# Order of weight splits and row preparation in an expert stage, and experts' weights read in 1 KB runs

## The reference

```
x = attention(x, state)                   # 8 batches x (512 + 32) tokens, 8 heads of 64: 4352 rows of 512
h = x @ w_in; x = (h * clip(h + 3, 0, 6) / 6) @ w_out          # 512 -> 2048 -> 512
logits = x @ w_gate; e_idx = argmax(logits, axis=1)
gate_w = softmax(logits)[e_idx]; eom = sigmoid(x @ w_output_gate)
for e in range(8):                        # w1[e]: 512 x 1024, w2[e]: 1024 x 512
    mask = e_idx == e
    out[mask] = gate_w[mask] * eom[mask, e] * (relu(x[mask] @ w1[e]) @ w2[e])
```

## Time and profile before

| | us |
|---|---|
| runs | 1163.8, 1163.85, 1164.52 |
| median | 1163.85 |
| the profiled execution's own time | 1164.95 |
| its span, first to last instruction | 1163.2 |

### The profile page before, as it was taken

How to read it: one execution, slowest core, us unless ns; L and a number is a source line. 1 busy time by engine, 2 the same in 40 slices (tenths; PEclk the granted TensorE clock), 3 DMA queues, 4 the chain that set the end, 5 groups by cost and what they waited for, 6 DMA issues and landing times.

```text
span 1163.2 us, 20924 instructions
## 1 busy us (share of the span) xinstructions
PE 1121.9 (96%) x6358; PEld 887.6 (76%) x6359; DVE 647.1 (56%) x1247; ACT 467.9 (40%) x781; POOL 76.8 (7%) x96
## 2 busy tenths in 40 slices
PE   9999999999999999999999988988899999989996
PEld 7777777777777777777778977867788888767885
DVE  6675654655646556556564347464465445446642
ACT  4454434443444344434544352442343223334420
POOL 0000100101001001010010110000101110000111
PEclk9999999999999999999999988989999999989998
DMA  9200110102001111020020275765676553765552
GB/s 365 91 37 8 66 37 37 44 30 74 37 6 68 37 37 41 33 74 1 1 110 1 104 252 179 244 208 176 218 236 208 163 160 117 243 203 177 178 155 63
DMA packets 98784, 131.37 MB, mean 113 GB/s; under 512 B 13967, under 2 KB 75023, under 8 KB 94352
## 3 DMA queue, kind: packets, MB, share of 16 engines
q1 hardware_dynamic: 91360, 89.35, 24.0%
q10 hardware_dynamic: 1584, 23.07, 5.9%
q0 software_dynamic: 5760, 17.90, 4.1%
HBM read 85.86 MB, written 45.47 MB: 113 GB/s over the span
## 4 chain that ended last, share of the span: by engine, by line
PE 80%; DVE 4%; DMA 4%; issue 3%; ACT 3%; SPq 3%; ACTq 2%; DVEq 0%; POOL 0%; POOLq 0%
PE y_ps L855 33%; PE h_ps L837 15%; PE y_ps L928 12%; PE h_ps L912 5%; PE y_ps L912 5%; DMA hid_mv<-hidden 3%; PE a_ps L812 2%; PE h_ps L827 2%; ACTq L444 2%; ACT we L1076 1%; DVE we L483 1%; SPq L574 1%; SPq L609 1%; PE a_ps L715 1%; PE a_ps L796 1%
## 5 line engine op out<-in xcount | busy, mean ns | idle before, releaser
L855 PE MATMUL y_ps<-w_out_hi,hid_hi 128*128 128x512 f32 x544 | 217.6, 400 | 0.0
L855 PE MATMUL y_ps<-w_out_hi,hid_lo 128*128 128x512 f32 x544 | 212.2, 390 | 0.0
L855 PE MATMUL y_ps<-w_out_lo,hid_hi 128*128 128x512 f32 x544 | 212.0, 390 | 0.0
L928 PE MATMUL y_ps<-we,act_t_hi 128*128 (+1 forms) x608 | 187.1, 389 | 1.2 <-DVE yo L1543 1.2
L1365 DVE SCALAR_TENSOR_TENSOR hid<-hid,h_ps 128x512 f32<-128x512 f32 (+1 forms) x144 | 94.4, 656 | 166.5 <-ACT hid L1035 166.5
L837 PE MATMUL h_ps<-att_hi,mix 128*128 128x512 f32 x512 | 184.0, 402 | 0.1
L1035 ACT ACTIVATE hid<-h_ps,three 128x512 f32<-128x512 f32 (+1 forms) x144 | 95.4, 662 | 174.9 <-PE h_ps L837 151.5
L855 PEld LDWEIGHTS y_ps<-w_out_hi,hid_hi 128*128 128x128 f32 x544 | 102.1, 188 | 50.0 <-issue 30.4
L1374 DVE TENSOR_TENSOR hid_lo<-hid,hid_hi 128x512 fp32r<-128x512 f32 (+1 forms) x144 | 94.8, 658 | 70.4 <-ACT hid_hi L1043 69.9
L928 PEld LDWEIGHTS y_ps<-we,act_t_hi 128*128 128x128 f32 x608 | 114.1, 188 | 25.2 <-issue 1.6
L912 PE MATMUL h_ps<-we,xg_t_hi 128*128 (+1 forms) x304 | 100.2, 413 | 22.8 <-DVE xg_t_lo L1419 11.5
(11 more groups left out here) (215 smaller groups left out, 1410.9 us busy)
## 6 DMA issues: line engine op xcount, KB each, us to landing
raw<-in_w ACTq DMA_DIRECT2D x11, 2048.0 KB, 8.3
hidden<-expert_hid SPq DMA_DIRECT2D x76, 256.0 KB
hid_mv<-hidden SPq DMA_DIRECT2D x152, 128.0 KB
xg<-buckets SPq DMA_DIRECT2D x164, 64.0 KB
xb<-in_x_rows SPq DMA_DIRECT2D x8, 1024.0 KB, 4.9
x_t<-in_x_t SPq DMA_DIRECT2D x7, 1024.0 KB, 4.9
buckets<-pad_row SPq DMA_DIRECT2D x8, 774.0 KB, 8.5
raw<-in_w SPq DMA_DIRECT2D x3, 2048.0 KB, 9.2
```

Of the source, the lines that this page charges most:

```text
L855: i = pe.matmul(y_ps[:, t, :], (hid_hi, hid_lo)[hp][:, hid_at(b, j), t * P:(t + 1) * P], w_out_s[wp][:, j, :], start=(j == 0 and m == 0), ...
L928: i = pe.matmul(y2_ps[:, slot % 2, :], act_t[hp][:, slot % 2, f, :], we[:, bass.ds(w_at + (wp * WPART + KD * F + f * DM), DM)], start=(f = ...
```

## The change

Three edits. The host lays w1 and w2 out as 16 pieces by 128 partitions by 256 floats, so that each of a load's 128 partition rows of 16 KB comes from 16 runs of 1 KB, 2048 runs in all; `by_pieces` gives the buffer the same shape. On DVE, the split of the first w2's pieces 1 to 3 in body 0 stands behind the rows of tile 2. And the w2 split stands ahead of `turn_hidden(t-1)` on DVE, and the w2 split with `load_w2` ahead of `hidden_hi(t-1)` on ACT.

```diff
-    F = w1.shape[3]
+    F = w1.shape[1] * w1.shape[3] * P // DM
...
+    def by_pieces(raw):
+        return raw[:].rearrange("p (i c) -> p i c", i=w1.shape[1])
...
-        sp.dma_start(raw1[:], w1[0].rearrange("p k f -> p (k f)")).then_inc(sem("raw1_loaded"), 16)
+        sp.dma_start(by_pieces(raw1), w1[0].rearrange("i p c -> p i c")).then_inc(sem("raw1_loaded"), 16)
...
-        sp.dma_start(raw2[:], w2[0].rearrange("p j d -> p (j d)")).then_inc(sem("raw2_loaded"), 16)
+        sp.dma_start(by_pieces(raw2), w2[0].rearrange("i p c -> p i c")).then_inc(sem("raw2_loaded"), 16)
...
-        sp.dma_start(raw1[:], w1[bass.ds(e, 1)].rearrange("o p k f -> p (o k f)")).then_inc(sem("raw1_loaded"), 16)
+        sp.dma_start(by_pieces(raw1), w1[bass.ds(e, 1)].rearrange("o i p c -> p (o i) c")).then_inc(sem("raw1_loaded"), 16)
         load_rows(Tile(0, 2))
...
         def load_w1(e, n):
             wait(act, "w1_ready", n)
-            act.dma_start(raw1[:], w1[bass.ds(e, 1)].rearrange("o p k f -> p (o k f)")
+            act.dma_start(by_pieces(raw1), w1[bass.ds(e, 1)].rearrange("o i p c -> p (o i) c")
                           ).then_inc(sem("raw1_loaded"), 16)
         def load_w2(e, n):
             wait(act, "w2_ready", n)
-            act.dma_start(raw2[:], w2[bass.ds(e, 1)].rearrange("o p j d -> p (o j d)")
+            act.dma_start(by_pieces(raw2), w2[bass.ds(e, 1)].rearrange("o i p c -> p (o i) c")
                           ).then_inc(sem("raw2_loaded"), 16)
...
             if not t.first:
-                hidden_hi(t.plus(-1))
                 if is_b(t.n, 1):
                     load_w2(entry(act, Tile(0, MT), T_NEXT, E - 1), 1)
...
                     split_hi(1, n, other)
                     with act.If(split2 > 1):
                         load_w2(entry(act, before_it, T_NEXT, E - 1), n + 1)
+                hidden_hi(t.plus(-1))
...
-            if t.first:
-                split_lo(dve, 1, 0, 0, range(1, PIECES), "w2_ready")
             with dve.If(split1 > 0):
                 split_lo(dve, 0, entry(dve, t, T_ORD, E - 1) + 1, entry(dve, t, T_OTHER, WSLOT), signal="w1_ready")
             if not (isinstance(t.n, int) and t.n + 2 >= MT):
                 turn_rows(t.plus(2))
                 rows_lo(t.plus(2))
+            if t.first:
+                split_lo(dve, 1, 0, 0, range(1, PIECES), "w2_ready")
             if not t.first:
+                before_it = t.plus(-1)
+                with dve.If(split2 > 0):
+                    split_lo(dve, 1, entry(dve, before_it, T_ORD, E - 1) + 1, entry(dve, before_it, T_OTHER, WSLOT),
+                             signal="w2_ready")
                 turn_hidden(t.plus(-1))
                 hidden_lo(t.plus(-1))
                 if not (isinstance(t.n, int) and t.n < LAG2):
                     put_out(t.plus(-LAG2))
-                before_it = t.plus(-1)
-                with dve.If(split2 > 0):
-                    split_lo(dve, 1, entry(dve, before_it, T_ORD, E - 1) + 1, entry(dve, before_it, T_OTHER, WSLOT),
-                             signal="w2_ready")
...
-    give("w1", inputs["moe2_w1"].reshape(E, 4, 4, 32, -1).transpose(0, 1, 3, 2, 4).reshape(E, 128, 4, -1))
+    give("w1", inputs["moe2_w1"].reshape(E, 4, 4, 32, -1).transpose(0, 1, 3, 2, 4).reshape(E, 128, 16, -1)
+         .transpose(0, 2, 1, 3))
-    give("w2", inputs["moe2_w2"].reshape(E, 2, 4, 4, 32, DM).transpose(0, 2, 4, 1, 3, 5).reshape(E, 128, 8, DM))
+    give("w2", inputs["moe2_w2"].reshape(E, 2, 4, 4, 32, DM).transpose(0, 2, 4, 1, 3, 5).reshape(E, 128, 16, -1)
+         .transpose(0, 2, 1, 3))
```

## The result

The changed kernel took 1158.45 us (median of 6 runs, 1156.05 to 1160.36), the kernel before, beside it, 1163.95 (6 runs, 1163.56 to 1165.67): 0.9947 of it, with a 95% interval of 0.9936 to 0.9959. It is faster by 5.5 us where the forecast, 1151, was 12.9 under the median shown. Its profiled execution took 1158.29, span 1156.5.

A forecast was written before the change was run, and what follows sets the result against it. TensorE, 96% busy, was taken to bound the kernel through gaps and slow clock in the expert stage. Gains and losses sum to 13.6 us; 1164.95 - 13.6 - 1.1 gives 1150.3, stated as 1151, range 1141 to 1175.

The forecast's parts named there:

- X: Time ACT is held by issuing one weight load of 2048 runs: taken as 1.5 us, range 0.35 to 4.2.
- hid_mv beside a load: Transfer returning a tile's hidden rows while a short-run weight load is in flight: 5.5 us, bounds 3.1 and 10.1.
- What bounds: TensorE is busy 96% of the span, so time can only come from its gaps and slow clock, together 32 us.
- f(28): First product of tile 28 in the expert stage: of 9.1 us lost there, 6.0 gained.
- the short runs don't spare hid_mv: Rival: hid_mv stays at 10 us beside a load, tile 28's first product keeps its gap; 1157 us, chance 0.13.
- Here alone the short runs are needed: At tile 28's first product: with hid_mv at 10 us the 6.0 us gain is lost.
- f(6): First product of tile 6: w2 split ahead of hidden in body 3 removes its loss, 6.7 us gained.
- f(10): First product of tile 10: body 7 repeats the earlier w2 split, 7.0 us gained.
- s(27): Second product of tile 27: hidden rows queue behind the w2 split's wait in body 28, 7.1 us lost.
- Tile 2's rows first: DVE order edit: tile 2's first product gains 3.0 + 2.8 us, but by itself the edit is worth nothing.
- f(4): First product of tile 4: 3.6 us idle and about 2.3 of clock come back, 5.9 lost.
- Held ACT: Rival: weight-load issues hold ACT, slower above 2.7 us each; 1166 to 1190 us, chance 0.25.

The follow-up runs named there:

- the version with the third value: Changed kernel, but for experts under three tiles w2's split and load stay behind the inner rows' split, flagged in the split column, one branch more: 1162.62 us, 0.9971.
- the one with the wait for `hid_moved`: Changed kernel with the w1 load behind the ReLUs and the w2 load behind hidden_hi and a wait for the transfer just issued: 1172.73 us, 1.0063.
- the version with SyncE's loads: Changed kernel, but loads from the third expert on are issued by SyncE right behind hid_mv, no longer by ScalarE: 1174.55 us, 1.0084.
- the w1 load behind the ReLUs: Kernel with only the 1 KB runs, both orders as before; w1's load issued after the step's two ReLUs, not ahead: 1146.13 us, 0.983.

## Why the prediction was off

**Sign right, size half, and the half by luck.** 13.6 us were forecast on the profiled execution, 6.7 came. Two errors of opposite sign stand in the sum, the issue time X and hid_mv beside a load.

**What bounds: right.** All that moved is gaps of the expert stage and the slow clock behind them. In the changed kernel the granted clock is 0.50 behind f(28)'s gap, as in the earlier trace rows:

```profile
1006.00:1012.00 6.00, 5.35 (x13) 0.50 0.48 134
```

**X: wrong, to the good side.** X was taken at 1.5 us, from w_in and hid_mv; it is 0.38 to 0.47. The forecast's own sum with that would have been 1145, so this error hid 6 us of the miss. A straight line from three rows of different DMAs to a fourth form didn't hold: 512 runs and 2048 runs took the same, and a single run of 1 KB took 0.48 to 0.73. The Trainium skill (Perfetto Trace Analysis, DMA Instruction, HWDGE) says that the descriptor generator is locked for an instruction until all its descriptors are made. That ScalarE would be held longer for more runs isn't seen here, and SyncE's four issues of hid_mv of tile 25, behind a load, took 2.56 us, as they do with no load near.

**The step that failed: "a load and a hid_mv that share turns should cost hid_mv some 2.5 us over its 3.08, so 5.5".** In the changed kernel hid_mv beside a load took 7.2 us at tiles 2 and 6, 7.7 at tile 24, and 8.3 to 9.2 at tiles 3, 7, 12 and 25. I had made it one number, a property of the run length. The experiments show it to be two: a load of 1 KB runs 0.3 to 0.6 us *behind* leaves hid_mv at 2.9 to 5.6, and the same load at the same moment or up to 4 us *ahead* makes it 7.0 to 9.8, where 16 KB runs ahead make it 7.1 to 8.6. In the changed kernel each hid_mv with the w2 load ahead landed within 1.6 us of that load. And it is the move that puts the load ahead. The next hid_mv waits for DVE's turn of the inner rows, and this turn now stands behind the w2 split, at whose end the load goes out: load of w2, turn, then hid_mv, 1.1 us later. Before, the w2 load went out after hid_mv of tile 25 had landed (1007.46 against 1004.1).

The trace before had one transfer in this order, which the prediction didn't use: with the first w2 load issued at 725.66, 3.1 us ahead of its last issue (728.77), hid_mv of tile 1 took 7.4 us (timeline, ACTq and SPq):

```profile
725.66 0.39 ACTq L1126 DMA_DIRECT2D raw<-in_w  x1
...
726.41 2.99 SPq L609 DMA_DIRECT2D hid_mv<-hidden  x4
```

The prediction had the pair of tile 25 in its text, "hid_mv of tile 25 goes out at 1001.0 beside the w2 load", and gave it 5.5 all the same. The rival "the short runs don't spare hid_mv", 1157, is the one that came nearest, given 0.13.

That one number carried f(28): +1.1 for +6.0, 4.9 of the 6.9 us missing. Of the 4.9, 2.7 are idle time and the rest slow clock, since the product behind the gap took 8.6 us here and 7.1 before, though the gap was shorter. With the load's bytes gone the gap is gone, and 8.1 us with it: 1.1 and 8.1 are 9.2, where the prediction's own working gives 8.9 for the true X (6.0 + 2.9). So its path to f(28) was right but for this term. The 1.67 at s(3), which isn't in the forecast, has the same cause: hid_mv of tile 3 took 8.95.

**"Here alone the short runs are needed": wrong.** At f(28) they did nothing for the moves (3.44 idle without them, 4.86 with them), and where the moves did need them, at s(0), the prediction had no wait. The moves and the short runs are two ways to the same waits, f(6), f(10) and f(28): each of those was a w2 split behind a late hid_mv. Short runs make hid_mv early (4.07 for 10.14), moves take the split out from behind it. The runs alone took the wait at f(6) and most of that at f(28), and left the one at f(10); the moves alone took those at f(6) and f(10) and half of that at f(28). Alone the runs give 12 us and the moves 5; together they give 5.5. Three things are shown to lie behind that: with the split out of the way an earlier hid_mv of tiles 2, 6 and 24 gained nothing (1160.01), the moves put the next load ahead of the next hid_mv (8.1 at f(28)), and they cost 7.1 at s(27), which the runs don't.

**Tile 2's rows first: right, worth nothing** in all three pairs. In the changed kernel f(4) gave back 3.5 and not 5.9, for there was no slow product behind its 3.21 idle. That is chance: in nine of the other versions f(4) took 7.3 to 8.6 us behind 2.9 to 4.4 idle, and 5.7 behind 3.1 in one. In the prediction, f(4) at 736.9 with 5.44 and 2.3 of clock ends at 744.6, not 744.2, so by its own times the edit loses 0.8 and not nothing. (And 1.2 + 0.6 + 0.8 in body 3 are 2.6, not 2.8; nothing hangs on it.)

**s(27): the mechanism right, the size by luck.** 7.1 for 7.1, ACT standing 15.03 us for s(26) in the row of 1031.82. But the forecast was 5.1 idle, 3.6 + X, and 2.0 of clock; measured are 4.35 idle and 2.8 of clock, and with the true X its rule gives 4.0 idle. The version with the third value gives 6.75 of it back.

**Held ACT: didn't occur.** It had 0.25 of the chances.

**Left open:** what the slow versions without a further read lost by their branch and what by waits, the one with the wait for `hid_moved` above all; why the product behind a gap of some 3 us is slow in one execution and not in another; and where the 1.3 us at the start of the stage and the 1.1 behind the last product come from.

## What to carry to other kernels

How long a small transfer takes beside a large one depends on which was issued first, so an edit that moves either must be priced with the order it makes; run length and order have to be tried one without the other, for here the layout alone gained twice what it gained with its companions. Put a large load a microsecond behind the small transfers that someone waits for, cut it into short runs, and look at the next transfer too, which may still meet it in flight. In a loop whose engines catch up after each stall, count reads of a table, and less so branches, as work of that chain.

## What of the hardware was not expected

- Issue on ScalarE or SyncE: a 2 MB load of 2048 runs of 1 KB 0.38 to 0.47 us, of 512 runs of 4 KB 0.38 to 0.46, of 128 runs of 16 KB 0.33 to 0.42; a single run of 1 KB 0.48 to 0.73. One exception isn't explained: the first w2 load of the version with SyncE's loads held ScalarE 2.45 us.
- Landing of ScalarE's loads: a median 12.3 us with 1 KB runs, 10.0 with 4 KB, 8.3 with 16 KB (page, part 6). Issued by SyncE, 2.1 to 2.7 us behind the last issue of a hid_mv, those of 1 KB runs landed in 8.4 to 8.8, so run length alone doesn't make the 12.3.
- hid_mv, 1024 runs of 512 B, took 2.7 to 4.9 us with no load near, median 3.2, over all versions. The table has it beside a load, by offset:

| the load | 2.6 to 4.1 us ahead | -0.4 to +0.2 | +0.2 to +0.6 | +0.7 and more |
|---|---|---|---|---|
| 1 KB runs | 7.9 to 9.8 | 7.0 to 9.0 | 2.9 to 5.6 | 2.7 to 4.8 |
| 4 KB runs | 8.6 | 8.4 to 10.0 | 6.4 to 10.2 | 2.9 to 3.5 |
| 16 KB runs | 7.1 to 8.6 | 9.3 to 12.0 | 9.0 to 11.4 | 2.8 to 3.1 |

- The last column is for transfers with no earlier load just ahead of them. With one issued 10.2 us before and in flight, hid_mv of tile 3 took 6.45 us at +1.2 (the w1 load behind the ReLUs); with one issued 12.3 us before, 7.8 at +0.8 (the runs alone).
- One read of a register from SBUF and one branch not taken: 1.04 us more between two operations on ScalarE, about 1 on VectorE; the branch alone 0.16. Over the kernel the pair on both engines cost 22 us.
